# Causal linear attention ahead of two gated layers: blocks of 64 tokens instead of 128 inside a chunk

## What is computed

```python
state = alpha[t][:, None] * state + outer(k[t], v[t]);  y[t] = q[t] @ state
x = y laid out as (3072 tokens, 384)
m = (sigmoid(x @ w_gate) * (x @ w_val)) @ w_out          # d_ff = 1536
out = max(m @ w1, m @ w2, m @ w3) @ w_out2               # d_ff = 768
```

## Time and profile before

| | us |
|---|---|
| median of 3 runs (859.74 to 861.74) | 861.67 |
| the profiled execution | 859.93 |
| its span, first to last instruction | 857.9 |
| TensorE busy (5653 matmul records) | 851.0 |
| VectorE busy | 364.2 |
| ScalarE busy | 279.2 |
| GpSimd busy | 75.9 |
| mean granted TensorE clock | 0.999 of full |

### The profile page before, as it was taken

The page is one execution under the profiler, slowest core; times in us unless marked ns, Lnnn a source line. Parts: engine busy times, 40 slices in busy tenths (PEclk is TensorE's granted clock), DMA queues, the critical chain, the costliest instruction groups (busy, mean ns, idle before and its releaser), DMA issues.

```text
span 857.9 us, 14194 instructions
## 1 busy us (share of the span) xinstructions
PE 851.0 (99%) x5653; PEld 790.4 (92%) x5653; DVE 364.2 (42%) x677; ACT 279.2 (33%) x520; POOL 75.9 (9%) x68
## 2 busy tenths in 40 slices
PE   8999999999999999999999999999999999999998
PEld 8899999999999999999999999988888888888887
DVE  8776554544454354374265232322323232232321
ACT  4555343333333333333333334421213122131312
POOL 1000111111021021021011004400000000000000
PEclk9999999999999999999999999999999999999999
DMA  7440210210210210201111023100100101010001
GB/s 282 171 169 3 99 47 2 100 47 2 99 47 2 99 47 2 87 17 44 49 51 47 7 74 112 37 1 1 37 1 1 37 0 37 0 37 0 20 17 38
DMA packets 14449, 42.14 MB, mean 49 GB/s; under 512 B 1984, under 2 KB 5952, under 8 KB 14400
## 3 DMA queue, kind: packets, MB, share of 16 engines
q1 hardware_dynamic: 14336, 41.38, 13.5%
q10 hardware_dynamic: 64, 0.05, 0.0%
HBM read 35.52 MB, written 4.72 MB: 47 GB/s over the span
## 4 chain that ended last, share of the span: by engine, by line
PE 97%; DVE 2%; issue 0%; ACT 0%; DMA 0%; ACTq 0%; DVEq 0%
PE ps_gv L915 35%; PE ps_out L940 18%; PE ps_gv L921 17%; PE ps_out L1034 6%; PE ps_sc L915 6%; PE ps_sc L921 3%; PE ps_pair L903 3%; PE ps_sc L866 2%; PE ps_pair L1034 2%; PE ps_pair L850 1%; PE ps_pair L899 1%; PE ps_sc L876 1%; DVE decay L629 0%; DVE rdec L641 0%; DMA inbuf<-att_in 0%
## 5 line engine op out<-in xcount | busy, mean ns | idle before, releaser
L915 PE MATMUL ps_gv<-x_hi,w_hi 128*128 128x384 f32 (+1 forms) x792 | 279.6, 353 | 1.1 <-ACT x_hi L404 1.1
L915 PE MATMUL ps_gv<-x_hi,w_lo 128*128 128x384 f32 (+1 forms) x792 | 277.1, 350 | 0.0
L921 PE MATMUL ps_gv<-x_lo,w_hi 128*128 128x384 f32 (+1 forms) x792 | 234.8, 350 | 0.0
L915 PEld LDWEIGHTS ps_gv<-x_hi,w_hi 128*128 128x128 f32 x792 | 148.7, 188 | 9.3 <-ACT w_hi L404 1.3
L915 PEld LDWEIGHTS ps_gv<-x_hi,w_lo 128*128 128x128 f32 x792 | 148.9, 188 | 7.5
L921 PEld LDWEIGHTS ps_gv<-x_lo,w_hi 128*128 128x128 f32 x792 | 146.0, 188 | 9.4
L719 DVE TENSOR_TENSOR h_sb<-act_sb,ps_gv 128x384 f32<-128x384 f32 x96 | 53.0, 552 | 164.1 <-PE ps_gv L921 163.5
L404 ACT ACTIVATE h_hi<-h_sb 128x384 fp32r<-128x384 f32 x96 | 50.4, 525 | 150.7 <-DVE h_sb L719 150.6
L450 ACT ACTIVATE act_sb<-ps_gv 128x384 f32<-128x384 f32 x96 | 47.2, 491 | 131.2 <-PE ps_gv L921 131.2
L816 DVE TENSOR_TENSOR probs<-probs,ps_gv 128x512 f32<-128x512 f32 x36 | 24.8, 689 | 137.9 <-PE ps_gv L921 137.9
L677 DVE TENSOR_TENSOR h_lo<-h_sb,h_hi 128x384 fp32r<-128x384 f32 x96 | 54.1, 564 | 52.0 <-ACT h_hi L404 52.0
(11 more groups left out here) (123 smaller groups left out, 973.7 us busy)
## 6 DMA issues: line engine op xcount, KB each, us to landing
inbuf<-att_in SPq DMA_DIRECT2D x23, 704.0 KB, 4.7
mid<-w SPq DMA_DIRECT2D x12, 576.0 KB, 8.4
inbuf<-att_in SPq DMA_DIRECT2D x23, 256.0 KB, 3.0
inbuf<-w SPq DMA_DIRECT2D x6, 768.0 KB, 4.3
out<-inbuf SPq DMA_DIRECT2D x5, 768.0 KB, 3.5
x_raw<-x_raw SPq DMA_DIRECT2D x46, 24.0 KB, 1.9
out<-inbuf SPq DMA_DIRECT2D x4, 192.0 KB, 2.0
mid<-att_in SPq DMA_DIRECT2D x1, 704.0 KB, 9.0
```

Of the source, the lines that this page charges most:

```text
L915: mm(bank, w_at(half, f, c + k * P, total=total), x_hi[:, k, 0:w], start=(k == 0 and half == 0), stop=False)
L921: return mm(bank, w_at(0, f, c + k * P, total=total), x_lo[:, k, 0:w], start=False, stop=(k == KT - 1))
```

## The change

From chunk 3 on, a chunk is worked in two blocks (s = 0, 1) of 64 tokens; chunks 0 to 2, in the prologue, stay whole. Scans run and restart per block. Scores are two 64 x 64 squares on the diagonal for each head, instead of one 128 x 128; block s writes rows 64s to 64s + 63 of the bank. The state is advanced twice per chunk (three state buffers instead of two), so the second block of a chunk is served by a state, also in the first chunk of a sequence. `outer` forms one sum per block (ps_sc, ps_sc_odd) and moves from f = 3c + 3 to f = 3c + 2, behind the value product; `new_state` moves to f = 3c + 2 on VectorE, behind h_rest. Of the value matmuls, the tokens of block s lie in row half s. Where the head's row half n equals s, they add to the same place as the state's; where it differs they go to `cross_bank(s)`, a place of their own, and VectorE adds them to x_raw afterwards (`y_add`, four operations, at f = 3c + 4, behind h_rest, ahead of scale_qk in tile 0). TensorE's scores and transposes, ScalarE's x_split(k = 0) and SyncE's move_last wait for y_added besides y_evac. SyncE's chunk loads wait for y_done where they waited for u_done. The constants get 64 more columns (a mask of 64 x 64, twice).

```diff
+SB = 64
+SUBS = CH // SB
...
+        def cross_bank(s):
+            lo = s * (512 + 2 * CH)
+            return ps_pair[:, lo:lo + 2 * SB].rearrange("p (a t) -> p a t", a=2)
...
             def move_last(T, parts=range(KT)):
...
                     sp.wait_ge(y_evac, CPT * (T + 1))
+                    sp.wait_ge(y_added, CPT * T)
...
             def scans(Cs, i):
...
                 for p in range(PAIRS):
-                    nc.vector.tensor_tensor_scan(decay[0:PR, par, p, :], att(buf(Cs), ALPHA)[:, p, :],
-                                                 zero[0:PR, :].broadcast_to([PR, CH]), 1.0, ALU.mult, ALU.add).then_inc(scan_done, 1)
+                    for s in range(subs(Cs, i)):
+                        t = span_of(Cs, i, s)
+                        nc.vector.tensor_tensor_scan(decay[0:PR, par, p, t], att(buf(Cs), ALPHA)[:, p, t],
+                                                     zero[0:PR, :].broadcast_to([PR, t.stop - t.start]), 1.0,
+                                                     ALU.mult, ALU.add).then_inc(scan_done, 1)
...
             def new_state(Cs, i):
...
                 dve.wait_ge(u_done, C + 1)
...
+                if not (isinstance(i, int) and Cs == 0):
+                    dve.wait_ge(y_done, C)
+                for s in range(subs(Cs, i)):
+                    next_state(Cs, i, s)
...
+            def y_add(Cs, i):
+                C, c = Cs + 6 * i, Cs % CPT
+                dve.wait_ge(y_evac, C + 1)
+                for n in range(2):
+                    at, u = slice(2 * n, 2 * n + 2), span_of(Cs, i, 1 - n)
+                    for r in HALVES:
+                        x = x_raw[r, at, c * CH + u.start:c * CH + u.stop]
+                        if Cs % (2 * CPT) == 0 and n == 1:
+                            ins = nc.vector.tensor_copy(x, cross_bank(0)[r, :, :])
+                        else:
+                            ins = nc.vector.tensor_tensor(x, x, cross_bank(1 - n)[r, :, :], ALU.add)
+                ins.then_inc(y_added, 1)
...
              def layer1(Ts, i, att_next, hooks):
...
-                    done = (C0 + c - 1, i) if att_next and f % 3 == 0 and c > 0 else None
...
-                    if done:
-                        new_state(*done)
+                    if att and f % 3 == 2:
+                        new_state(*att)
+                    if att_next and f % 3 == 1 and c > 0:
+                        y_add(C0 + c - 1, i)
...
             def scores(Cs, i):
...
                     pe.wait_ge(y_evac, C)
-                    pe.wait_ge(state_done, C)
+                    if not (isinstance(i, int) and Cs == CPT):
+                        pe.wait_ge(y_added, C - CPT)
+                    pe.wait_ge(state_done, states_by(Cs, i) - SUBS)
+                w = CH // subs(Cs, i)
...
-                    for r, bank in zip(HALVES, score_banks(Cs, i)):
-                        ins = mm(bank[:, p * CH:(p + 1) * CH], att(buf(Cs), K, r)[:, p, :],
-                                 att(buf(Cs), Q, r)[:, p, :], start=True, stop=True)
+                    for s in range(subs(Cs, i)):
+                        t = span_of(Cs, i, s)
+                        for r, bank in zip(HALVES, score_banks(Cs, i)):
+                            ins = mm(bank[t, p * w:(p + 1) * w], att(buf(Cs), K, r)[:, p, t],
+                                     att(buf(Cs), Q, r)[:, p, t], start=True, stop=True)
...
             def outer(Cs, i):
...
                 pe.wait_ge(khs_done, C + 1)
+                if not (isinstance(i, int) and Cs < CPT):
+                    pe.wait_ge(mask_done, 2 * C + 2)
...
+            def value(Cs, i, p, n, s, start=False):
+                t = span_of(Cs, i, s)
+                if subs(Cs, i) == 1 or n == s:
+                    to = y_slot(Cs, i, p, n, s)
+                else:
+                    to = cross_bank(s)[HALVES[(p + n) % 2], p // 2, :]
+                return mm(to, v_cols(buf(Cs), (2 * p + n) * D, D)[t, :],
+                          probs_of(Cs, i)[t, PAIRS * n + p, :], start=start, stop=True, skip_group_check=True)
...
             def layer1(Ts, i, att_next, prev, hooks):
...
+                    if att_next and f in (2, 5, 8):
+                        outer(C0 + (f - 2) // 3, i)
                     if att_next and f in (3, 6, 9):
                         attend(C0 + (f - 3) // 3, i)
-                        outer(C0 + (f - 3) // 3, i)
```

More of the change, by code:

```diff
@@ new lines, in new_state, with next_state @@
+                for s in range(subs(Cs, i)):
+                    next_state(Cs, i, s)
+            def next_state(Cs, i, s):
+                j = state_at(Cs, i, s)
+                past = states_by(Cs, i) - subs(Cs, i) + s
+                old, new = state[0:PR, j], state[0:PR, (j + 1) % 3]
+                u = outer_bank(Cs, i, s)[0:PR, :].rearrange("p (a e) -> p a e", a=PAIRS)
+                last = span_of(Cs, i, s).stop - 1
+                end = decay[0:PR, Cs % 2, :, last:last + 1].broadcast_to([PR, PAIRS, D])
+                if Cs % (2 * CPT) == 0 and s == 0:
+                    nc.vector.tensor_tensor(new, u, end, ALU.mult).then_inc(state_done, 1)
+                else:
+                    dve.wait_ge(state_done, past)
+                    nc.vector.tensor_tensor(stmp[0:PR], u, old, ALU.add).then_inc(stmp_done, 1)
+                    dve.wait_ge(stmp_done, states_by(Cs, 0) - subs(Cs, i) + s - Cs // (2 * CPT) + (6 * SUBS - 1) * i)
+                    nc.vector.tensor_tensor(new, stmp[0:PR], end, ALU.mult).then_inc(state_done, 1)
@@ L891, in attend @@
                     pe.wait_ge(y_evac, C)
[L892 to L895 removed]
+                    pe.wait_ge(state_done, states_by(Cs, i))
+                else:
+                    if Cs == 2:
+                        pe.wait_ge(y_evac, 1)
                     pe.wait_ge(state_done, C)
+                for s in range(1 if first else 0, subs(Cs, i)):
                     for p in range(PAIRS):
                         for n, r in enumerate(HALVES):
[L899 to L905 removed]
+                            mm(y_slot(Cs, i, p, n, s), state[r, state_at(Cs, i, s), p, :],
+                               att(buf(Cs), Q, r)[:, p, span_of(Cs, i, s)],
+                               start=(p < 2 and s == (1 if first else 0)), stop=False, skip_group_check=True)
+                if subs(Cs, i) == 1:
+                    for p in range(PAIRS):
+                        for n in range(2):
+                            ins = value(Cs, i, p, n, 0, start=(first and p < 2))
+                else:
+                    for p in range(PAIRS):
+                        for n in range(2):
+                            value(Cs, i, p, n, n)
+                    for p in range(PAIRS):
+                        for n in range(2):
+                            ins = value(Cs, i, p, n, 1 - n, start=True)
                 ins.then_inc(y_done, 1)
@@ L1008, in _ @@
             outer(1, 0)
-            unused(10, ident, mask)
+            unused(10, ident, ident)
             scores(2, 0)
@@ L1165, in lay_out @@
     consts[:, P:2 * P] = np.triu(np.ones((P, P)))
+    consts[:, 2 * P + 4:] = np.tile(np.triu(np.ones((SB, SB))), (SUBS, 1))
     consts[0:D, 2 * P] = 1
```

131 lines of the change are left out of this document (67 added, 64 removed).

## The result

| | before | after |
|---|---|---|
| median of 4 runs, us | 861.1 (859.74 to 861.74) | 866.93 (865.73 to 868.6) |
| ratio | | 1.0077, 95% interval 1.0059 to 1.0094 |
| profiled execution, us | 859.93 | 865.73 |
| its span | 857.9 | 863.7 |
| start of TensorE's last matmul | 854.54 | 859.10 |

The changed kernel is slower by 0.8%, beyond the 0.3% that can be told from no change. The forecast was 862.3 in a range of 851 to 871: the range holds, the sum (+0.6) was 5 us short. The four runs of the changed kernel also differ in their mean granted clock: 865.73 and 866.36 us at 0.999 and 1.0, 867.5 and 868.6 at 0.998 and 0.995.

What follows compares the result with a forecast made beforehand. The prediction took TensorE, busy 851.0 of 857.9 us, to bound the kernel. Its terms, -12.8 + 9.5 + 2.4 + 1.5 = +0.6 us, on the median of 861.67 gave 862.3, range 851 to 871.

Steps and rivals of the forecast that it cites:

- The saving: TensorE's attention matmuls run in quarters of the array: -0.66 us for 18 chunks, -0.30 for 3, -12.8 us in all.
- The issue-bound rival: Matmuls in quarters cannot start more often than every 0.0224 us: +10 in place of -12.8, 885 us; chance 0.08.
- The boundary's mechanism and place: At 7 tile boundaries SyncE's row moves wait for y_added at f = 10, delaying x's third part 1.35 us: +9.5.
- one gap of 1.2 us: Sign: at each boundary TensorE shows one gap of about 1.2 us before x's third part, released by ScalarE's x_hi.
- the cover of 0.55 us: At f = 5 and 8, y_add would end 0.55 us before the scores need it, so it hides in the tiles.
- if score matmuls wait for y_added in every chunk: Sign that the forecast is wrong: TensorE's scores waiting for VectorE's y_add in every chunk.
- y_add stands ahead: 2 x 0.76: In tile 0, y_add at f = 4 and 7 precedes VectorE's scaling of q and k, without cover: +1.5 us.
- the load behind the moves: The next chunk's alpha, queued behind SyncE's row moves, lands late at 6 boundaries: +2.4 us (0 to 4).
- The rival in which the chunk load decides: Late chunk loads hold the first value product after f = 0 at 6 boundaries: +8, 870 us; chance 0.19.
- The prologue's chunks stay whole: 0: In the prologue nothing is lost: its chunks stay whole and the constants' extra 32 KB have cover, 0 us.
- as forecast: Whole run: a sum near zero of terms of some 13 us on each side, 858 to 866 us; chance 0.54.
- the boundary stays hidden: Rival: the moves and loads at tile boundaries land in the cover, leaving -11.3, 850.4 us; chance 0.19.

Runs made afterwards that it cites:

- order: The changed kernel with all score matmuls of block 0 first, then all of block 1, so consecutive ones use two quarters of the array: 874.26 us, ratio 1.0149.
- add_f9: The changed kernel with only the y_add of a tile's third chunk moved from f = 10 to f = 9: 854.84 us, ratio 0.9929.
- old_wait10: The kernel before, with SyncE's move_last also waiting for h_lo of f = 10, nothing else changed: 864.83 us, ratio 1.0046.
- scale_first: The changed kernel with only q and k of tile 0 scaled ahead of h_rest at f = 4 and 7: 867.29 us, ratio 1.0081.
- old_wait_h11: The kernel before, with SyncE's move_last held until h_sb of f = 11: 902.7 us, ratio 1.0497.
- early_pro: The changed kernel with y_add at f = 3, 6, 9 and the prologue's splits of x ahead of chunk 3's backward scans: 850.04 us, ratio 0.9874.
- best: early_pro with q and k of tile 0 scaled ahead of h_rest at f = 4 and 7: 847.93 us, ratio 0.9856.
- after_pad: The changed kernel with 24 always met waits on SyncE ahead of the last four output DMAs: 868.26 us, ratio 1.0096.
- add_early: The changed kernel with every y_add one step sooner, at f = 3, 6, 9: 852.44 us, ratio 0.9898.
- no_add: The changed kernel without y_add and its waits, so y lacks half of the attention's values: 850.09 us, ratio 0.9874.

## Why the prediction was right and where it failed

**Right.** That TensorE bounds, so that every change on it counts in full. The saving: -12.8 forecast, -13.4 measured, with the slot of 0.058 for 64 columns from the line through 0.045 and 0.109; `order` shows that it needs the alternation of quarters. That the sum came this close has some luck in it: states and values saved 0.45 and not 0.53 a chunk, and the outer products' move cost 0.23 and not 0.34. Issue costed at nothing: four matmuls start from 261.55 to 261.57, as close as the earlier trace rows had them. By the 25 ns between starts that the Trainium skill gives (TensorE: Matmul & The Clock Gate, section "Wait — 56ns, not 53.3ns?"), an estimate for the 32 scores is 0.8 us; they are 0.48, so for quarters of the array the trace disagrees. The issue-bound rival is refuted. The boundary's mechanism and place, the new wait on SyncE, released as foretold: add_f9 removes it, old_wait10 makes it in the kernel before. One sign was read too simply: there is not one gap of 1.2 us ahead of the third part of x, but 0.58 ahead of the second and 0.47 ahead of the third.

**Mis-sized: y_add.** The working took four operations of 0.27 overlapping by 0.08, 0.84 us, from scans and from operations of 192 and 384 elements. The four take 1.18. The source view of the changed kernel (ns min/median/max):

```profile
L736 DVE TENSOR_TENSOR x_raw<-x_raw,ps_pair x78: 272/286/294, 54.8 to 498.1; 48x128 f32<-48x128 f32 x78
```

One is near the 0.27, but they follow each other at 0.30: the overlap that the four scans have was carried over to operations that show none. The 0.34 decides three terms. It is most of what the boundary has over the forecast (1.71 for 1.35, 12.0 for 9.5). It takes 0.34 of the cover of 0.55 us for the scores at f = 5 and 8. And it lengthens tile 0's waits.

**Left out: the way from y_add to the scores.** The cover was counted from y_add's end to the start of the scores, as if the way between them took nothing; it takes 0.36 us, since two more waits stand behind the one for y_added on TensorE. 0.55 - 0.34 - 0.36 = -0.15, the wait that was measured, 12 times. Either term alone was covered. The point that the working gave, 0.41 us an operation, left this way out. The working's sign of being wrong, "if score matmuls wait for y_added in every chunk", came true at 12 of 21 chunks. To put the wait for y_added last of the three would, as an estimate from the two steps of 0.11, take the 0.15 away; no run has tried it.

**Mis-sized: tile 0.** "y_add stands ahead: 2 x 0.76" is 1.25 each. k decides both waits, and it comes 1.21 later than before against the gate product of f = 5: y_add's whole 1.18, with no 0.08 off for overlap, and not 0.84 less 0.08. The scores' other edge, y_added, lies hidden behind k and shows only in scale_first.

**Over-sized: the load behind the moves.** +2.4 forecast, +0.4 measured, nearly all in tile 3. Alpha does land late (the scans at 302.65 waited only 0.18 for it, then ran on), but h_sb is ready in time in most tiles, the delay of the gate product giving it the room. The rival in which the chunk load decides had 870 from this place, and its mechanism is absent. A loss beyond the gap itself can come for another reason, as old_wait_h11 shows: the clock.

**Missed: the prologue.** "The prologue's chunks stay whole: 0". Chunks 0 to 2 do, but chunk 3 is the first halved one and its scans are written into the prologue, ahead of the split of x: a late alpha (scans begin 0.9 us later than before, although its load was issued no later, 21.65 for 21.84 us; why it lands late is open), forward scans 1.56 for 1.37 and backward 2.03 for 1.60. I costed that extra scan time, and placed it "in the tiles". 1.5 us; early_pro takes it back.

**Missed: the tail**, +1.3, on no step of the forecast, cause open.

So the verdict came from a sum of large terms of both signs in which most errors went to one side: 8.1 us too little (boundary 2.5, scores 1.8, prologue 1.5, tail 1.3, tile 0 1.0), against 2.6 the other way (load 2.0, saving 0.6). That the range holds the result is owed to its width: the case "as forecast" ended at 866, and the case whose time lies next above, 870, has a mechanism that the trace does not show. The time of the rival "the boundary stays hidden" (850.4) was reached once the additions were placed well, early_pro 850.04, best 847.93, though with other small terms in the sum.

## What to carry to other kernels

When a change trades work on the bounding engine for work elsewhere, list every place at which the new operation stands ahead of something that was just in time, the last step of a tile and the prologue above all, and ask there for the earliest step at which its inputs exist. Here that is one step earlier, and it was worth 14 of the 19 us between the changed kernel and the best one. An overlap or a price is taken from rows of the same operands (PSUM against SBUF, few against many partitions), a cover is counted to the moment at which the waiting engine can start and not to the last instruction's end, and where it is thinner than the error of these prices, it is not cover. If a wait has two causes, take away both before judging either.

## What the runs showed that I had not expected

- VectorE's additions of 48 x 128 from PSUM take 0.286 us each and follow at 0.30, with no overlap, where eight scans of 64 elements take 1.56 together.
- Matmuls of 64 columns in one quarter start 0.058 us apart whether neighbours use two quarters or four; what the order decides is how many quarters are busy at once: 32 matmuls start within 0.477 us if they alternate over four, within 0.758 if they take two and then the other two.
- A wait costs TensorE time even behind the one that decides: with the waits for the state and for k behind the one for y_added, each 0.11 us after the last, a score starts 0.36 us after y_add's end; where the wait for k decides and is the last, it starts 0.15 after k.
- A gap in TensorE's stream can cost more than its length: with 2.18 + 0.6 us at a boundary the clock fell to 0.50 every time and added some 1.5 us a boundary (10.6 over seven) to 4.1 expected. The length of the gap alone does not decide: in the prologue, waits of 1.42, 1.61 and 1.77 us (changed kernel, add_f9, scale_first) left it at 1.00, waits of 1.56, 1.57, 1.63 and 1.72 (after_pad, order, add_early, no_add) were followed by 0.50.
- An always met wait on SyncE, idle there, costs the run nothing (ratio 1.000), but a DMA issue on it can take 1.0 to 1.7 us instead of 0.37 when a packet of its instructions moves in the same moment; at the end of a kernel nothing hides it.
